# Attention with pooled queries and a channel mix: a ring of eleven places for the forms of tokens, and another place for the turned tiles

## The reference, cut to what matters

```python
# q, k, v: (4, 8, 1152, 64)
q_pool = q.reshape(B, H, S // 2, 2, D).mean(axis=3)          # 576 pooled queries
scores = scale * q_pool @ k^T;  scores -= max                # softmax over 1152 keys
attn = exp(scores) / (sum(exp(scores)) + 1e-09)
x = (attn @ v), heads side by side                           # (4, 576, 512)
# channel mix
mu, var = mean(x), var(x) over the last axis
xn = (x - mu) / sqrt(var + 1e-06) * g_ln
out = x + max(xn @ w_ch1, 0) @ w_ch2                         # 512 -> 2048 -> 512
```

## Time and profile before

| | |
|---|---|
| time before, median of 3 runs | 822.96 us (822.94 to 823.75) |
| the profiled execution's own time | 822.77 us |
| its span, first to last instruction | 820.1 us |
| PE busy | 798.5 us (97%) |
| DVE busy | 645.6 us (79%) |
| ACT busy | 417.3 us (51%) |
| POOL busy | 458.1 us (56%) |
| granted TensorE clock, mean | 0.995 |
| DMA moved | 75.35 MB, mean 92 GB/s |

### The profile page before, as it was taken

The page is one execution under the profiler, slowest core; times in us unless marked ns, Lnnn a source line. Parts: engine busy times, 40 slices in busy tenths (PEclk is TensorE's granted clock), DMA queues, the critical chain, the costliest instruction groups (busy, mean ns, idle before and its releaser), DMA issues. The chain is left out here.

```text
span 820.1 us, 17078 instructions
## 1 busy us (share of the span) xinstructions
PE 798.5 (97%) x6488; PEld 668.1 (81%) x6488; DVE 645.6 (79%) x984; ACT 417.3 (51%) x941; POOL 458.1 (56%) x347
## 2 busy tenths in 40 slices
PE   8999999999999999999999999998999997999998
PEld 6777777787777777677778999978989987899997
DVE  6798889888889999888457866798886789867655
ACT  4676556576556576665824335443244443433431
POOL 3988888888889888797793311353321236122100
PEclk9999999999999999999999999999999999999999
DMA  8566444566544456311112212113322111421212
GB/s 190 126 144 144 117 89 107 120 145 144 123 89 104 117 144 144 87 53 30 31 53 65 89 53 64 52 52 118 102 66 89 52 53 52 141 91 52 65 39 77
DMA packets 39680, 75.35 MB, mean 92 GB/s; under 512 B 8880, under 2 KB 23472, under 8 KB 36016
## 3 DMA queue, kind: packets, MB, share of 16 engines
q1 hardware_dynamic: 38128, 73.88, 34.4%
q10 hardware_dynamic: 1472, 0.39, 0.3%
HBM read 69.54 MB, written 4.72 MB: 91 GB/s over the span
## 5 line engine op out<-in xcount | busy, mean ns | idle before, releaser
L563 POOL TENSOR_TENSOR acc<-acc,pT 128x576 f32<-128x576 f32 x160 | 238.3, 1489 | 23.2 <-ACT pT L895 0.4
L1250 PE MATMUL banks<-w2f,hT 128*128 128x512 f32 x864 | 213.7, 393 | 0.0
L895 ACT ACTIVATE pT<-banks 128x576 f32<-128x576 f32 x288 | 171.8, 653 | 36.9 <-PE banks L695 31.5
L1240 PE MATMUL banks<-xf,w1f 128*128 128x384 f32 x924 | 179.9, 342 | 8.4 <-DVE mid L1404 8.4
L1250 PEld LDWEIGHTS banks<-w2f,hT 128*128 128x128 f32 x864 | 160.6, 188 | 28.3 <-issue 0.2
L1005 DVE TENSOR_REDUCE pm<-banks 128x2 f32<-128x1024 f32 x128 | 153.2, 1221 | 37.8 <-PE banks L641 36.6
L1240 PEld LDWEIGHTS banks<-xf,w1f 128*128 128x128 f32 x924 | 166.4, 191 | 17.1 <-issue 10.4
L697 PE MATMUL banks<-qT,kT 64*128 64x288 f32 x1728 | 162.2, 298 | 3.5 <-DVE pm L1005 2.3
L697 PEld LDWEIGHTS banks<-qT,kT 64*128 64x128 f32 x1728 | 133.6, 184 | 18.8 <-DVE pm L1005 7.5
L708 PE MATMUL banks<-pT,vn 128*64 128x288 f32 x1152 | 145.9, 407 | 0.0
L1328 ACT ACTIVATE hT<-mid 128x384 fp32r<-128x384 f32 x88 | 46.2, 527 | 189.1 <-DVE mid L1404 188.3
(11 more groups left out here) (114 smaller groups left out, 882.2 us busy)
## 6 DMA issues: line engine op xcount, KB each, us to landing
q_in_rows<-in_q_dram SPq DMA_DIRECT2D x56, 284.0 KB, 6.8
k_in_rows<-in_k_dram SPq DMA_DIRECT2D x56, 284.0 KB, 5.2
w_stage<-in_moe_w_ch_dram SPq DMA_DIRECT2D x24, 512.0 KB, 3.9
w_stage<-in_moe_w_ch_dram SPq DMA_DIRECT2D x48, 256.0 KB, 2.7
vn<-in_v_dram SPq DMA_DIRECT2D x16, 576.0 KB, 5.0
out_dram<-x SPq DMA_DIRECT2D x16, 256.0 KB, 3.3
q_in_rows<-in_q_dram SPq DMA_DIRECT2D x4, 256.0 KB, 3.0
k_in_rows<-in_k_dram SPq DMA_DIRECT2D x2, 288.0 KB, 4.2
```

The source lines that it names most:

```text
L563: nc.gpsimd.tensor_tensor(total, pT[:, h % 2, 0] if kt == 1 else total, pT[:, h % 2, kt], ALU.add).then_inc(chained, 1)
L895: nc.scalar.activation(pT[:, h % 2, kt], pair_banks("S", n)[:, :, 0:HW], ACT.Exp, scale=SCALE).then_inc(exp_done, 1)
L1240: last = nc.tensor.matmul(banks[:, PRODUCT_BANK[i], 0:CW], w1f[:, m % W_RING, a, c], xf[:, i, b, c], start=at == 0, stop=at == len(terms) - 1)
L1250: last = nc.tensor.matmul(banks[:, k % 2 * (CT // 2) + kk], hT[:, k, a, tokens], w2f[:, (2 * u + k // 2) % 4, b], start=p == 0 and k < 2 a ...
```

## The change

Eleven places instead of seven hold the forms of tokens: `xf` keeps its seven, and `xf_more` adds four, which lie on memory that only the first stage uses. Form i of part n has place (7n + i) mod 11. `form_free` waits for the product that last read the place: for part 1 the first four forms have new places and the last three wait for products 0 to 2 of unit 7; for part 2 likewise.

The preparation of the next part is moved forward by a unit: four statistics in the tail of p = 1, the last two, the mean and the variance within p = 2 (behind the low part of hidden tile 0, ahead of V5), normalized tiles at the tails of p = 2, 3 and 4 and within p = 4 and 5, turned tiles in p = 3, 4 and 5. The forms are made in p = 4 (B11), 5 (B21), 6 (T1, T2) and 7 (T3, B22, T4): high parts on ACT, and all low parts on DVE, in one place of the unit, behind the low part of hidden tile 2. POOL makes the sums T1 and T2 at the start of p = 6 and T3 and T4 at the start of p = 7, and no low part.

In `PAIR_STEPS` the two T of a pair, which stood behind PV@2 in banks 1 and 0, are parted: the first stands ahead of PV@2 in bank 4, the second behind it in bank 0.

```diff
--- before.py
+++ after.py
@@ -53,6 +53,7 @@
...
     W_RING = 9
+    X_RING = 11
     PLAIN = 2
...
@@ -81,7 +82,7 @@
...
     PAIR_STEPS = ("M@4 S@6 S@2 S@0 M@4 S@6 S@2 M@0 S@6 M@4 S@2 S@0 S@6 M@2 S@4 S@0 S@6 S@4 M@0 S@2 S@6 M@4 S@0 M@2 "
-                  "S@6 M@4 S@0 O@6 E@3 L@0 PV@2 T@1 T@0 KQ@4 KA@6 SH@3 Z@1 PV@0")
+                  "S@6 M@4 S@0 O@6 E@3 L@0 T@4 PV@2 T@0 KQ@4 KA@6 SH@3 Z@1 PV@0")
     PAIR_END = PAIR_STEPS[:PAIR_STEPS.index("O@6")] + "O@6 E@3 Z@5 PV@2 E@3 O@6 PV@0"
...
@@ -208,6 +209,7 @@
...
             w2f = sb("w2f", [128, 4, 2, DM], f32r, mix)
+            xf_more = sb("xf_more", [128, X_RING - FORMS, 2, HC, CW], f32r, mix)
...
@@ -335,6 +337,24 @@
...
+        def token_form(n, i):
+            at = (FORMS * n + min(i, T4)) % X_RING
+            return xf[:, at] if at < FORMS else xf_more[:, at - FORMS]
+        def form_free(eng, n, i):
+            before = FORMS * n + i - X_RING
+            if before >= 0:
+                eng.wait_ge(product_done, products_before(FP * (before // FORMS + 1) - 1) + before % FORMS + 1)
+            elif n:
+                eng.wait_ge(down_done, 1)
+            elif i == T4:
+                eng.wait_ge(product_done, products_before(PLAIN))
         def tokens_hi(eng, copy, n, i):
...
@@ -342,17 +362,13 @@
...
                 eng.wait_ge(tokens_summed, 4 * n + (T1, T2, T3, T4).index(i) + 1)
-            if n:
-                eng.wait_ge(product_done, products_before(FP * n - 1) + i + 1)
-            elif i == T4:
-                eng.wait_ge(product_done, products_before(PLAIN))
-            copy(xf[:, min(i, T4), 0], token_source(i)).then_inc(x_hi[i], 1)
+            form_free(eng, n, i)
+            copy(token_form(n, i)[:, 0], token_source(i)).then_inc(x_hi[i], 1)
...
             vector.wait_ge(x_hi[i], n + 1)
-            at = min(i, T4)
-            eng.tensor_tensor(xf[:, at, 1], token_source(i), xf[:, at, 0].bitcast(f32),
-                              ALU.subtract).then_inc(x_lo[i], 1)
+            form = token_form(n, i)
+            eng.tensor_tensor(form[:, 1], token_source(i), form[:, 0].bitcast(f32), ALU.subtract).then_inc(x_lo[i], 1)
...
@@ -1127,13 +1143,16 @@
...
             n, p = divmod(u, FP)
-            return [(n + 1, kk) for kk in range(2 * p - 8, 2 * p - 6)] if 4 <= p < 7 and n + 1 < PARTS else []
-        def at_border(u):
+            return [(n + 1, kk) for kk in range(2 * p - 6, 2 * p - 4)] if 3 <= p < 6 and n + 1 < PARTS else []
+        def forms_made_in(u):
...
             n, p = divmod(u, FP)
-            return n + 1 if p == FP - 1 and n + 1 < PARTS else None
+            return {4: (B11,), 5: (B21,), 6: (T1, T2), 7: (T3, B22, T4)}.get(p, ()) if n + 1 < PARTS else ()
+        def sums_made_in(u):
+            return [i for i in forms_made_in(u) if i in (T1, T2, T3, T4)]
...
@@ -1178,21 +1197,12 @@
...
             for u in range(1, UNITS):
-                n = at_border(u)
-                if n:
-                    sum_tokens(nc.gpsimd, pool, n, T1)
-                    sum_tokens(nc.gpsimd, pool, n, T2)
-                if behind_border(u):
-                    tokens_lo(nc.gpsimd, pool, u // FP, T3)
-                    tokens_lo(nc.gpsimd, pool, u // FP, T4)
+                for i in sums_made_in(u):
+                    sum_tokens(nc.gpsimd, pool, u // FP + 1, i)
                 if u + 2 < UNITS:
...
                     inverse_deviation(u // FP + 1)
-                if n:
-                    sum_tokens(nc.gpsimd, pool, n, T3)
-                    sum_tokens(nc.gpsimd, pool, n, T4)
-                    tokens_lo(nc.gpsimd, pool, n, B22)
...
@@ -1210,7 +1220,7 @@
...
                     last = nc.tensor.matmul(banks[:, 6 + b, 0:CW], w1f[:, (m + half) % W_RING, ap, c],
-                                            xf[:, ((B11, B21), (T4, B22))[b][half], bp, c], start=at == 0,
+                                            token_form(0, ((B11, B21), (B12, B22))[b][half])[:, bp, c], start=at == 0,
                                             stop=at == len(terms) - 1)
...
@@ -1357,12 +1368,8 @@
...
             for u in range(PLAIN, UNITS):
-                n, turns = at_border(u), turned_in(u)
+                turns = turned_in(u)
                 first_copy(u)
-                if n:
-                    tokens_hi(act, nc.scalar.copy, n, B11)
-                if behind_border(u):
-                    tokens_hi(act, nc.scalar.copy, u // FP, T3)
                 if u == PLAIN:
...
@@ -1370,23 +1377,18 @@
...
                 next_hi(u, 1, 2)
-                if n:
-                    tokens_hi(act, nc.scalar.copy, n, T2)
-                    tokens_hi(act, nc.scalar.copy, n, B21)
-                if behind_border(u):
-                    tokens_hi(act, nc.scalar.copy, u // FP, T4)
                 next_hi(u, 2, 4)
                 second_hi(2 * u)
-                if n:
-                    tokens_hi(act, nc.scalar.copy, n, T1)
+                for i in forms_made_in(u)[:2]:
+                    tokens_hi(act, nc.scalar.copy, u // FP + 1, i)
                 hidden_hi(u, 1)
...
                 second_hi(2 * u + 1)
-                if n:
-                    tokens_hi(act, nc.scalar.copy, n, B22)
+                for i in forms_made_in(u)[2:]:
+                    tokens_hi(act, nc.scalar.copy, u // FP + 1, i)
                 hidden_hi(u, 3)
...
@@ -1430,20 +1432,29 @@
...
                     return
-                if p in (1, 2):
+                if p == 1:
                     dve.wait_ge(x_written, PAIRS)
-                    for kk in range(CT // 2):
-                        statistics(n, CT // 2 * (p - 1) + kk)
+                    for kk in range(4):
+                        statistics(n, kk)
                 if p == 2:
+                    normalize(n, 0)
+                    normalize(n, 1)
+                if p == 3:
+                    normalize(n, 2)
+                if p == 4:
+                    normalize(n, 4)
+            def next_tokens_within(u):
+                n, p = u // FP + 1, u % FP
+                if n == PARTS:
+                    return
+                if p == 2:
+                    statistics(n, 4)
+                    statistics(n, 5)
                     moments_of(n)
                     variance_eps(n)
-                if p == 3:
-                    normalize(n, 0)
-                    normalize(n, 1)
-                if p == 4:
-                    normalize(n, 2)
-                if p == 5:
-                    normalize(n, 4)
+                if p in (4, 5):
+                    normalize(n, 2 * p - 5)
...
@@ -1459,20 +1470,17 @@
...
             for u in range(PLAIN, UNITS):
-                n = at_border(u)
                 middle(u, "V")
-                if n:
-                    tokens_lo(nc.vector, dve, n, B11)
                 next_lo(u, 0, 1)
...
                     tokens_lo(nc.vector, dve, 0, T4)
-                if u // FP + 1 < PARTS and u % FP in (5, 6):
-                    normalize(u // FP + 1, 2 * (u % FP) - 7)
+                if u % FP in (4, 5):
+                    next_tokens_within(u)
                 next_lo(u, 1, 2)
                 hidden_lo(u, 0)
-                if n:
-                    tokens_lo(nc.vector, dve, n, T2)
+                if u % FP == 2:
+                    next_tokens_within(u)
                 middle(u, "V5")
...
@@ -1483,9 +1491,8 @@
...
                 hidden_lo(u, 2)
-                if n:
-                    tokens_lo(nc.vector, dve, n, B21)
-                    tokens_lo(nc.vector, dve, n, T1)
+                for i in forms_made_in(u):
+                    tokens_lo(nc.vector, dve, u // FP + 1, i)
                 if behind_border(u):
...
```

More of the change, by code:

```diff
@@ L1240, in product @@
                     last = nc.tensor.matmul(banks[:, PRODUCT_BANK[i], 0:CW], w1f[:, m % W_RING, a, c],
-                                            xf[:, i, b, c], start=at == 0, stop=at == len(terms) - 1)
+                                            token_form(u // FP, i)[:, b, c], start=at == 0,
+                                            stop=at == len(terms) - 1)
                 last.then_inc(product_done, 1)
```

## The result

The changed kernel takes **812.38 us** (median of 4 runs, 811.98 to 815.0) against 822.98 us of the kernel before in the same series (822.94 to 823.75): ratio 0.9876, 95% interval 0.9854 to 0.9898. The forecast was 810.8, the range 808.0 to 816.0.

A forecast was written before the change was run, and what follows sets the result against it. PE's own work plus waits for DVE's sums at the borders, held up by POOL, bounded the kernel. Gains of 14.9 us less additions of 1.0 and 1.7 gave -12.2, so 810.8 us; 8-in-10 range 808.0 to 816.0.

The forecast's parts named there:

- the case that had the chance of 0.70: The forecast's own case for the whole kernel's time: 808.8 to 813.5 us.
- The stall of units 8 and 16 goes: Units 8 and 16: POOL's low parts leave the border, T3 and T4 are summed earlier; -5.58 and -5.83 us.
- Units 7 and 15: B11 and T2 no longer between sums of products, -0.78 and -0.59 us; V late behind POOL's sums, +0.5 us each.
- The row sums: Pairs 12, 13 and 14: with the first turned tile in bank 4, row sums wait for nothing new; -2.1 us.
- Units 2 and 10: Statistics, mean and variance ahead of V5 delay products 5 and 6: +1.2 and +0.5 us, bounds 0 and 5.
- Elsewhere nothing: Rest of the kernel: tiles, ACT copies, sums of weights and a part's outputs were to cost nothing more.
- The rival that had the stall come a unit earlier: Units 7 and 15 each lose 2.1 us more by one more held-up DVE instruction; 815 us, chance 0.14.
- The half-open border: Product 3 at the border still waits, for a late form; half the gain there, 818 us, chance 0.06.
- the slower case: The stall arises in both units of each border, 5.6 us in each of four; 832 us, chance 0.04.

The follow-up runs named there:

- experiment 2: The kernel before with only the ring of eleven places and the waits of `form_free`, all forms made where they were before: 824.02 us, ratio 1.0017.
- experiment 5: The kernel before with the low parts of T3, T4 and B22 moved from POOL to DVE, no ring, no earlier unit: 817.7 us, ratio 0.9943.
- experiment 7: The kernel of experiment 4 with the low parts of T1 and T2 ahead of 12 in units 6 and 14: 809.38 us, ratio 0.984.
- experiment 1: The kernel before with only the first turned tile of a pair moved to bank 4, ahead of the values: 820.33 us, ratio 0.9967.
- experiment 4: The changed kernel with the last two statistics, mean and variance of p = 2 behind the second weights' low part, not ahead of V5: 810.15 us, ratio 0.9848.
- experiment 6: The changed kernel with the buffers `w2f` and `xf_more` in each other's place in memory: 811.85 us, ratio 0.9871.
- experiment 9: The kernel of experiment 5 with B22's low part moved from unit 7's tail into the border unit beside T4's: 817.47 us, ratio 0.9939.
- experiment 3: The changed kernel with T3's and B22's low parts on POOL in unit 7 and T4's at unit 8's start: 813.43 us, ratio 0.9891.

## Why the prediction was right

The time came out 1.6 us above the forecast, inside its range, in the case that had the chance of 0.70. Step by step (units from product 0 to product 0):

1. *The stall of units 8 and 16 goes.* Right, and well sized: 15.68 and 15.64 us are left of 21.16 and 21.41, so -5.5 and -5.8, as forecast. V of unit 8 starts 548.72 - 544.05 = 4.7 us in, the forecast's figure. The cause that the step named is shown by the runs: with eleven places and POOL's row of four unchanged the stall stays (experiment 2), and with two of the four gone and their low parts made by DVE, nothing else moved, it shrinks, though only to 19.39 and 19.29 us (experiment 5). The rest goes in the changed kernel, with the two sums a unit earlier and the three low parts behind them.
2. *and 4. Units 7 and 15.* V was forecast at +7.3 and came at 534.95 - 527.82 = +7.1. The unit takes 16.23 where the two steps together gave 16.36 - 0.78 + 0.5 = 16.1. Unit 15 takes 16.22. One DVE instruction per POOL instruction was the right price, and it was T2's low part that came first: POOL's sum of T3 started at 528.68 beside it and took 2.43 us instead of 1.90. Experiment 7 takes both sums away from the tail, and the pauses go.
3. *The row sums.* -2.1 forecast; unit 2 starts 2.2 us earlier, and the step alone gives 2.5 (experiment 1).
5. *Units 2 and 10.* Right in place, too small in size. 1.2 and 0.5 were forecast. Unit 2 takes 17.47 us, 1.9 more than before; unit 10 takes 16.65, 1.07 more, of which 0.1 is the surplus of `xf_more`. Together 2.9 instead of 1.7, within the stated bounds. V5 came at +11.8 and +11.3, half a us behind the forecast's +11.3 and +10.8. The parts of that sum were less good than the sum: in unit 10 the fourth statistic in the tail, priced at 0.6, put V off by less than 0.1 (+5.33 against +5.25), while POOL's sums of weights lengthened two instructions by 1.1; the forecast's start of V5 had no term for them, only the loss of PE had been rounded up. Experiment 4, which moves this work alone, gains 2.2. The size is not the same in every execution: in the profiled run of experiment 6, where this work has the same order, the two units took 17.14 and 17.48 us.
6. *Elsewhere nothing.* This step failed: the products that read `xf_more` and the down tiles beside them cost 1.2 us that no wait shows. The trace of before has no such buffer and could not show it, and a bound above nothing should have stood there, since the change gives PE a new buffer to read.

The sum: of the span's forecast fall of 12.2 us 9.8 came. 1.2 of the rest is step 5, 1.2 step 6, and the other steps were off by 0.2 or less each and cancelled. The profiled execution's time outside the span happened to be 1.0 lower, which the forecast held constant and which hid part of the miss; that was luck, since it differs as much between two runs of one kernel.

The rival that had the stall come a unit earlier, with one more held-up instruction, did not happen: two are held up, by two sums. The Trainium skill (SBUF — State Buffer, Who interferes with whom) has whoever starts first hold the shared ports for the whole instruction, and says that a VectorE instruction with at most one SBUF input, outside its two-port modes, does not contend. The rows agree with both: the two `mid` of experiment 7 keep their 0.5 us each within POOL's 2.44 us, while the two `hT` behind them, with both operands in SBUF, take 3.19 for both where 1.2 is usual (1.23 in the same place of the changed kernel, at 526.44). The half-open border did not happen either: no form is late. Nor did the slower case: unit 8's V stands early.

## What to carry to other kernels

Where two engines hold each other up, price the block by how many instructions of the one stand in a row beside the other's urgent ones, not by the work moved: two sums beside a tail cost 0.4 us, four cost 3.7 and then the clock. The count is the price, but when the row ends decides whether anybody pays it (times from product 0 of the unit; product 3 stands at 7.3):

| | POOL's row | it ends | V starts | PE's pause before product 3 |
|---|---|---|---|---|
| before, unit 8 | 4 | +9.9 | +10.5 | 3.74 |
| experiment 5, unit 8 | 2 | +6.3 | +8.1 | 1.36 |
| experiment 9, unit 8 | 2 | +5.7 | +7.2 | 0.46 |
| changed, unit 7 | 2 | +5.3 | +7.1 | 0.40 |
| experiment 3, unit 8 | 3 | +4.2 | +6.4 | none |
| experiment 7, unit 7 | 2 | +2.8 | +5.4 | none |

A piece that is moved must be priced where it lands (the statistics ahead of V5, B22 beside the sums of weights), and when one wait is taken away the next consumer of the same engine is to be looked at first. More room in memory gains nothing by itself; it gains by what it allows to be done earlier, here ahead of a stretch in which all forms fell due at once.

## What the runs showed of the hardware that was not expected

- Down tiles beside products that read the second buffer of tokens take 2.08 us for their nine matmuls instead of 2.05, with no wait, at two different addresses. It is in the ring alone, too: in experiment 2 such a tile lasts from 742.83 to 744.91, again 2.08. The cause is open; no kernel was run in which a single buffer holds all eleven places.
- The same pause does not always cost the same behind it. In experiment 2 PE stood still for 4.14 us before product 3 of unit 16, and the granted clock was 0.63 over the next 7.9 us; in the kernel before it stood still for 4.16 us there, and the clock was 0.79 over the next 7.3. Unit 16 lasted 22.65 us against 21.41.
- In experiment 5 pauses of PE of 1.36 and 0.38 us were followed by a granted clock of 0.79 and then 0.68 over 6.4 us. The pauses of 0.3 to 0.9 us in the changed kernel left it at 1.00, and so did the one of 1.71 in experiment 9, with 0.46 and 0.37 ahead of it (1.00 over the 4.4 us behind it), so the length of the pause alone does not settle it.
